# Joins, norm sums and roots moved between places of a hand-written order: attention by chunks, a maxout layer and a routed expert layer on one core

## The chip, the cores and the metric

One core of a Trainium2 chip runs the whole program. The metric is device microseconds of one execution. The engines are TensorE (PE, with its weight loads PEld), VectorE (DVE), ScalarE (ACT), GpSimd (POOL) and SyncE (SP), which here only issues DMAs. Each engine takes its instructions in the order in which the program issues them, and waits on semaphores that the others raise.

## The reference, cut to what matters

There are three stages, one after the other. The inputs are `q, k, v, a_re, a_im` of 4 x 8 x 768 x 48.

```python
mag = np.sqrt(a_re * a_re + a_im * a_im)
scale = np.minimum(mag, 0.999) / (mag + 1e-06)
a_re_n, a_im_n = (a_re * scale, a_im * scale)
for t in range(S):
    ar, ai = (a_re_n[:, :, t, :, None], a_im_n[:, :, t, :, None])
    new_re = ar * S_re - ai * S_im
    new_im = ar * S_im + ai * S_re
    kv = np.einsum('bhd,bhe->bhde', k[:, :, t], v[:, :, t])
    S_re, S_im = (new_re + kv, new_im)
    y[:, :, t] = np.einsum('bhd,bhde->bhe', q[:, :, t], S_re)
...
h = np.maximum(np.maximum(x @ w1, x @ w2), x @ w3)      # x: 3072 x 384, w: 384 x 768
x2 = h @ w_out
...
# each token of x2 goes to one of 8 experts by cosine with expert_emb:
out[mask] = gate_w[mask, None] * (np.maximum(x2[mask] @ e1[e], 0.0) @ e2[e])
```

## The kernel before, in words

**Chunks and pairs.** The 3072 tokens are 24 chunks of 128 (NC = 24), six to a batch. Two chunks make a pair g (12 pairs). For a pair the running products of the complex decay `a` are needed. They lie in one of four ring slots, and are made in this order: the decay is normalised in two halves m = 2g and 2g+1 (24 "norms"); GpSimd multiplies along blocks of 16 steps (`chain_steps(g, 1..15)`); VectorE joins the four blocks with three `join(g, b)`; GpSimd takes the pair's end for the state (`turns(g)`); ScalarE copies the pair's products into `z_t` (`stage_z(n)`), once for each chunk. Pair 0 is made by VectorE alone, in blocks of eight with seven joins. Pairs 0 and 1 come from memory directly. From pair 2 on a norm's result is stored to a scratch in memory, and loaded back from there into the ring (`store_unit`, `load_ring` on SyncE).

**One norm** is passed between ScalarE and VectorE: `norm_square` (ACT, L663), `norm_m2` (DVE, L1032), `norm_mag` (ACT, two activations, L668 and L670), `norm_sum` (DVE, L1037), `norm_rsqrt` (ACT, three activations, L674, L676, L679), `norm_inverse` (DVE, two operations, L1052 and L1054), `norm_rest` (ACT, L689), `norm_apply` (DVE, two operations, L1059 and L1062). There is one tile for the squares of all norms, so `norm_square(m)` waits for `norm_m2(m-1)`.

**The chunk loop** stands once for each engine, as an order written out by hand. In round n TensorE makes the scores of chunk n (L1627), turns its keys (L1637), adds to the state (L1648) and makes the answers (L1660, L1668). Among these it makes, for chunk n-1, the six groups of nine matmuls of the maxout layer (`moe_up`, `mm` of L1570, L1571, L1574), and for chunk n-2 the transposes of h and the product with `w_out` (`moe_ht`, `moe_down`). Its order in a round is: half the scores, `moe_ht(n-2, 0)`, the other scores, group 0, `moe_ht(n-2, 1)`, `moe_down(n-2)`, keys, group 1, state, group 2, answers, groups 3 to 5. Group 0 needs `x_hi` (ACT, L741) and `moe_max(n-2, 1, 1)`; group 3 needs `moe_max(n-1, 0, 1)`, group 4 `moe_max(n-1, 0, 2)`, group 5 `moe_copy(n-1, 1)` (ACT, L735). The scores of chunk n+1 need `k_decay(n+1)` (L1178).

VectorE prepares the next chunk in the same round: `z_norm(n+1)` (L1152), after ScalarE's `z_square(n+1)` (L709); `z_newton(n+1)` (two operations, L1159 and L1161), after ScalarE's `z_recip(n+1)` (two activations, L714 and L716); then `q_decay` and `k_decay`. Among these stand the maxima (`moe_max`, L1109), the mask (L1121), the state's turn (`rotation`, L1131 to L1136), `add_state` (L1146), the joins (four operations each, L1089 to L1093) and the norms. Which norms and joins a round has is set by `norms_in`, `joins_early` and `joins_late`.

ScalarE's order in a round is: `moe_x_hi(n-1)`, `moe_h_hi(n-2, 0)`, the square of a second norm, `stage_z(n+1)`, `moe_h_hi(n-2, 1)`, `z_square(n+1)`, `moe_copy(n-1, 0)`, `moe_out`, `kp_copy(n)`, `z_recip(n+1)`, all `norm_mag`, all `norm_rsqrt`, the next norm's square, `y_copy(n)`, `moe_copy(n-1, 1)`, all `norm_rest`. With `late_z` the staging stands after `kp_copy`.

After chunk 23 come the routing and the 30 expert tiles, which the change doesn't touch.

## Time and profile before

| | |
|---|---|
| median of 3 runs | 990.97 us (989.76 to 991.07) |
| the profiled execution | 990.71 us |
| its span, first to last instruction | 989.0 us |
| mean granted TensorE clock | 0.943 of full |
| busy share of the span | PE 88%, PEld 78%, DVE 66%, POOL 50%, ACT 47% |
| chain that ended last | PE 52%, DVE 17%, POOL 11%, ACT 6%, issue 5%, DMA 5%, SPq 2% |

Between the span and the profiled execution's time lie 1.7 us of start and end. The granted clock has two levels, full (2.4 GHz) and half (1.2 GHz); a value between them is a mean over a stretch that had both. The chunk loop takes the stretch from 65 to 645 us.

### The profile page before, as it was taken

To read this page: it belongs to the slowest core of one execution; us is meant where nothing else is said; L and a number is where in the kernel's file an instruction comes from. 1 tells how busy PE (TensorE), PEld (TensorE's weight loads), DVE (VectorE), ACT (ScalarE), POOL (GpSimd) and SP (SyncE) were. 2 spreads that over 40 slices of the span, in tenths; PEclk is the share of its full clock that TensorE was granted. 3 is DMA by queue.
4 is the path that set the end of the run, shared out by engine and by line. 5 is a ranking of instruction groups with operands and counts; after the bars stand their busy time and mean duration, and the time that the engine had idled before them with its cause. 6 is when DMAs were issued, how large, how long until landed. Compare 5 with 4: busy or idle time off the path is not lost.

```text
span 989.0 us, 18419 instructions
## 1 busy us (share of the span) xinstructions
PE 873.7 (88%) x6398; PEld 776.1 (78%) x6399; DVE 656.4 (66%) x1054; ACT 461.2 (47%) x859; POOL 491.1 (50%) x888
## 2 busy tenths in 40 slices
PE   0568887999989999999999999839999999999995
PEld 0445777888878898889889888838888888888785
DVE  5968677898799989999876755267323252556721
ACT  5765635555555566565344442233222242446521
POOL 1290998199998989889791000023222222223221
PEclk9767889999989999999999999967999999999998
DMA  9204232542414243331321110334411151416311
GB/s 302 65 20 106 73 81 68 139 106 71 118 53 112 87 118 87 93 86 54 87 64 40 38 46 19 139 137 167 168 40 40 40 168 40 167 34 210 121 40 32
DMA packets 42247, 90.80 MB, mean 92 GB/s; under 512 B 6312, under 2 KB 23728, under 8 KB 40768
## 3 DMA queue, kind: packets, MB, share of 16 engines
q1 hardware_dynamic: 38080, 77.48, 26.1%
q0 software_dynamic: 4096, 12.40, 4.0%
q8 instruction: 41, 0.67, 0.3%
q14 instruction: 30, 0.25, 0.1%
HBM read 70.20 MB, written 18.48 MB: 90 GB/s over the span
## 4 chain that ended last, share of the span: by engine, by line
PE 52%; DVE 17%; POOL 11%; ACT 6%; issue 5%; DMA 5%; SPq 2%; DVEq 0%; ACTq 0%; POOLq 0%
PE mm L1570 6%; PE mm L1574 5%; PE mm L1571 5%; PE yu L1570 4%; PE tr L1570 4%; PE tr L1571 4%; PE tr L1574 4%; PE yu L1571 4%; PE yu L1574 4%; POOL c_im L1889 3%; PE mm L1808 3%; POOL c_re L1888 3%; POOL ring L1891 2%; POOL ring L1892 2%; PE sc L1627 2%
## 5 line engine op out<-in xcount | busy, mean ns | idle before, releaser
L1570 PE MATMUL mm<-up_hi,x_hi 128*128 128x384 f32 x432 | 160.0, 370 | 34.2 <-DVE h_sb L1109 12.1
L1888 POOL TENSOR_TENSOR c_re<-ring 112x128 f32<-112x128 f32 x165 | 102.4, 620 | 108.0 <-DMA ring<-an_scratch 60.1
L1571 PE MATMUL mm<-up_lo,x_hi 128*128 128x384 f32 x432 | 149.9, 347 | 0.0
L1966 POOL DMA_INDIRECT out_rows<-g_o,rows_out x30 | 34.7, 1155 | 182.0 <-DVE g_o L1487 182.0
L1570 PEld LDWEIGHTS mm<-up_hi,x_hi 128*128 128x128 f32 x432 | 83.5, 193 | 50.6 <-DVE h_sb L1109 15.5
L952 ACT ACTIVATE g_h<-tr 128x512 f32<-128x512 f32 x60 | 35.8, 597 | 171.6 <-PE tr L1574 166.1
L1889 POOL TENSOR_TENSOR c_im<-ring 112x128 f32<-112x128 f32 x165 | 109.3, 662 | 0.0
L1574 PE MATMUL mm<-up_hi,x_lo 128*128 128x384 f32 x432 | 101.8, 345 | 0.0
L1891 POOL TENSOR_TENSOR ring<-c_re,c_im 112x64 f32<-112x64 f32 x165 | 83.8, 508 | 12.9
L1892 POOL TENSOR_TENSOR ring<-c_re,c_im 112x64 f32<-112x64 f32 x165 | 86.8, 526 | 0.0
L1109 DVE TENSOR_TENSOR h_sb<-mm,h_sb 128x384 f32<-128x384 f32 x96 | 52.9, 551 | 48.5 <-PE mm L1574 46.4
L1571 PEld LDWEIGHTS mm<-up_lo,x_hi 128*128 128x128 f32 x432 | 84.2, 195 | 0.0
L1478 DVE TENSOR_TENSOR gh_lo<-mm,gh_hi 128x512 fp32r<-128x512 f32 x60 | 41.4, 691 | 63.3 <-ACT gh_hi L960 60.8
L1570 PE MATMUL yu<-e_hi,gh_hi 128*128 (+1 forms) x240 | 83.0, 346 | 0.1
L1574 PEld LDWEIGHTS mm<-up_hi,x_lo 128*128 128x128 f32 x432 | 81.2, 197 | 0.0
L1571 PE MATMUL yu<-e_lo,gh_hi 128*128 (+1 forms) x240 | 80.9, 337 | 0.0
L1570 PE MATMUL tr<-e_hi,gx_hi 128*128 (+1 forms) x180 | 72.9, 405 | 2.0 <-DVE e_lo L1347 1.4
L1571 PE MATMUL tr<-e_lo,gx_hi 128*128 (+1 forms) x180 | 72.3, 402 | 0.0
L1627 PE MATMUL sc<-q_t,k_t 48*128 48x128 f32 x768 | 60.7, 303 | 11.5 <-DVE k_t L1178 9.1
L1627 PEld LDWEIGHTS sc<-q_t,k_t 48*128 48x128 f32 x768 | 51.5, 205 | 22.0 <-issue 22.0
L1347 DVE TENSOR_TENSOR e_lo<-raw,e_hi (+2 forms) x40 | 56.0, 1434 | 9.6 <-ACT e_hi L940 9.6
L1487 DVE TENSOR_SCALAR g_o<-yu,table_gate 128x384 f32 (+1 forms) x30 | 18.5, 618 | 63.9 <-PE yu L1574 63.3
(242 smaller groups left out, 2093.2 us busy)
## 6 DMA issues: line engine op xcount, KB each, us to landing
raw<-in_moe_w SPq DMA_DIRECT2D x16, 1536.0 KB
a_dn<-in_a_laid SPq DMA_DIRECT2D x20, 384.0 KB, 7.2
an_scratch<-a_dn SPq DMA_DIRECT2D x20, 384.0 KB, 2.3
ring<-an_scratch SPq DMA_DIRECT2D x20, 384.0 KB, 6.2
q_in<-in_q_laid SPq DMA_DIRECT2D x24, 224.0 KB, 3.0
k_in<-in_k_laid SPq DMA_DIRECT2D x24, 224.0 KB, 3.2
v_in<-in_v_laid SPq DMA_DIRECT2D x24, 192.0 KB, 3.3
x_scratch<-x_sb SPq DMA_DIRECT2D x24, 192.0 KB, 2.7
```

Of the source, the lines that this page charges most:

```text
L952: nc.scalar.activation(g_h[:, half * FREE:(half + 1) * FREE], tr[:, half, :], ACT.Relu) \
L1109: nc.vector.tensor_tensor(hh, mm[:, (3 * half + w) % 2, 0:FH], hh, ALU.max).then_inc(p_maxed, 1)
L1347: nc.vector.tensor_tensor(flat(lo), flat(raw), flat(hi).bitcast(F32), ALU.subtract).then_inc(expert_lo, 1)
L1478: nc.vector.tensor_tensor(gh_lo[:, part, :], mm[:, half, :].rearrange("p (k t) -> p k t", t=P), gh_hi[:, part, :].bitcast(F32), ALU.subtra ...
L1570: nc.tensor.matmul(out, hi[:, x, :], w_hi(x), start=(x == 0), stop=False)
L1571: nc.tensor.matmul(out, hi[:, x, :], w_lo(x), start=False, stop=False)
L1574: last = nc.tensor.matmul(out, lo[:, x, :], w_hi(x), start=False, stop=(x == K - 1))
L1627: last = nc.tensor.matmul(sc[:, b, h * P:(h + 1) * P], k_t[rows, x, h, :], q_t[n % 2][rows, x, h, :], start=(x == 0), stop=(x == 1))
L1888: nc.gpsimd.tensor_tensor(c_re[:, 0:count, :, :], cur, bc(prev[:, :, 0, :], 2, 2), ALU.mult).then_inc(chain_prod, 1)
L1889: nc.gpsimd.tensor_tensor(c_im[:, 0:count, :, :], cur, bc(prev[:, :, 1, :], 2, 2), ALU.mult).then_inc(chain_prod, 1)
L1891: nc.gpsimd.tensor_tensor(cur[:, :, 0, :], c_re[:, 0:count, 0, :], c_im[:, 0:count, 1, :], ALU.subtract).then_inc(chain_step, 1)
L1892: nc.gpsimd.tensor_tensor(cur[:, :, 1, :], c_re[:, 0:count, 1, :], c_im[:, 0:count, 0, :], ALU.add).then_inc(chain_step, 1)
```

## The change

It moves work within the orders of ScalarE and VectorE; no arithmetic is added or left out.

- Norm 10 goes from chunk 3 to chunk 4, which so has norms 10 and 11.
- Pair 2's joins: the first from ahead of `z_norm(3)` in chunk 2 to the end of that chunk, the second the same way into chunk 3, and the third from the end of chunk 2 into chunk 3. Pair 5's first join goes from the end of chunk 7 into chunk 8.
- In chunk 3 ScalarE stages chunk 4's products after `kp_copy`, as it does in chunk 1.
- In chunk 1 the state's turn and the second norm's first step stand behind the joins.
- `norm_sum` of every chunk goes ahead of `z_newton` and `moe_max(n-1, 0, 2)`.
- Norms 4 and 5, ahead of the loop and in chunk 0: their first steps, magnitudes and sums come earlier, their roots are apart, and their inverses stand between the scalings of chunk 0.

```diff
--- before.py
+++ after.py
@@ -472,16 +472,18 @@
 
             if n == 0:
                 return ()
-            first = 6 if n == 1 else n + 6 if n < 4 else n + 7
-            count = 2 if n in (1, 3) else 1
+            first = 6 if n == 1 else n + 6 if n < 5 else n + 7
+            count = 2 if n in (1, 4) else 1
             return tuple(m for m in range(first, first + count) if m < NORMS)
 
         joins_early = {1: [(1, b) for b in range(NBLK - 1)]}
         joins_late = {}
-        for g in range(DIRECT, NG):
-            joins_early[2 * g - 2] = [(g, 0), (g, 1)] if g < 5 else [(g, 1)]
+        joins_late[2] = [(2, 0)]
+        joins_early[3] = [(2, 1), (2, 2)]
+        for g in range(3, NG):
+            joins_early[2 * g - 2] = [(g, 0), (g, 1)] if g < 6 else [(g, 1)]
             joins_late[2 * g - 2] = [(g, 2)]
-            if g >= 5:
+            if g >= 6:
                 joins_late[2 * g - 3] = [(g, 0)]
 
         def router_bank(r):
@@ -831,19 +833,19 @@
             split_dn()
             norm_square(4, norm_of(4))
             low_copy(range(4, 8))
+            norm_square(5, norm_of(5))
+            norm_mag(4, norm_of(4))
             stage_z(0)
             z_square(0)
-            norm_square(5, norm_of(5))
+            norm_mag(5, norm_of(5))
             z_recip(0)
-            norm_mag(4, norm_of(4))
-            norm_mag(5, norm_of(5))
             low_copy(range(8, 12))
 
             for n in range(NC + 2):
                 prev, prev2, now, more = 1 <= n <= NC, n >= 2, n < NC, n + 1 < NC
                 norms = norms_in(n) if now else ()
                 later = norms_in(n + 1) if now else ()
-                late_z = n == 1
+                late_z = n in (1, 3)
                 if prev:
                     moe_x_hi(n - 1)
                 if prev2:
@@ -856,6 +858,8 @@
                     moe_h_hi(n - 2, 1)
                 if more and not late_z:
                     z_square(n + 1)
+                if n == 0:
+                    norm_rsqrt(4, norm_of(4))
                 if prev:
                     moe_copy(n - 1, 0)
                 if prev2:
@@ -866,13 +870,13 @@
                     kp_copy(n)
                 if n == 0:
                     low_copy(range(12, 14))
-                    norm_rsqrt(4, norm_of(4))
-                    norm_rsqrt(5, norm_of(5))
                 if more and late_z:
                     stage_z(n + 1)
                     z_square(n + 1)
                 if more:
                     z_recip(n + 1)
+                if n == 0:
+                    norm_rsqrt(5, norm_of(5))
                 for m in norms:
                     norm_mag(m, norm_of(m))
                 if n == 0:
@@ -1214,16 +1218,18 @@
             norm_apply(2, norm_of(2))
             first_chain(7)
             norm_apply(3, norm_of(3))
-            for number in range(7):
+            for number in range(4):
                 join(0, number)
             norm_m2(4, norm_of(4))
+            for number in range(4, 7):
+                join(0, number)
+            norm_m2(5, norm_of(5))
+            norm_sum(4, norm_of(4))
             z_norm(0)
-            norm_m2(5, norm_of(5))
+            norm_sum(5, norm_of(5))
             z_newton(0)
             q_decay(0)
             k_decay(0)
-            norm_sum(4, norm_of(4))
-            norm_sum(5, norm_of(5))
 
             for n in range(NC + 2):
                 prev, prev2, now, more = 1 <= n <= NC, n >= 2, n < NC, n + 1 < NC
@@ -1247,24 +1253,32 @@
                     moe_h_lo(n - 2, 1)
                 if now:
                     mask(n)
-                if now and n >= 1:
+                if now and n >= 2:
                     rotation(n)
-                for m in norms[1:]:
+                for m in norms[1:] if n >= 2 else ():
                     norm_m2(m, norm_of(m))
                 for g, number in joins_early.get(n, ()):
                     join(g, number)
+                if n == 1:
+                    rotation(n)
+                    for m in norms[1:]:
+                        norm_m2(m, norm_of(m))
                 if more:
                     z_norm(n + 1)
+                if n == 0:
+                    norm_inverse(4, norm_of(4))
                 if prev:
                     moe_max(n - 1, 0, 1)
                 if now:
                     add_state(n)
+                for m in norms:
+                    norm_sum(m, norm_of(m))
                 if more:
                     z_newton(n + 1)
                 if prev:
                     moe_max(n - 1, 0, 2)
-                for m in norms:
-                    norm_sum(m, norm_of(m))
+                if n == 0:
+                    norm_inverse(5, norm_of(5))
                 if more:
                     q_decay(n + 1)
                     k_decay(n + 1)
@@ -1273,8 +1287,6 @@
                 for m in norms:
                     norm_inverse(m, norm_of(m))
                 if n == 0:
-                    for m in (4, 5):
-                        norm_inverse(m, norm_of(m))
                     for m in (4, 5):
                         norm_apply(m, norm_of(m))
                 if prev:
```

## Rows read from the trace of the kernel before

**Rows 1.** The page: its first line, the span and the instructions.

```profile
span 989.0 us, 18419 instructions
```

**Rows 2.** By stretch: length, busy PE, PEld, DVE, ACT, POOL; clock, DMA share, GB/s.

```profile
114.77:148.12 33.35, 28.45 (x199) 25.61 (x199) 23.97 (x36) 12.93 (x26) 30.91 (x62) 0.75 0.37 99
148.12:176.44 28.32, 23.30 (x199) 20.83 (x199) 21.36 (x36) 16.97 (x34) 21.36 (x46) 0.94 0.19 60
176.44:202.73 26.29, 23.22 (x199) 20.52 (x198) 22.82 (x38) 12.38 (x26) 9.36 (x14) 0.94 0.52 132
202.73:224.47 21.74, 21.37 (x200) 19.54 (x199) 18.96 (x29) 13.57 (x27) 20.25 (x39) 0.99 0.49 121
224.47:269.04 44.57, 41.13 (x365) 37.03 (x365) 37.68 (x58) 25.23 (x51) 41.66 (x76) 1.00 0.36 95
269.04:319.26 50.22, 45.07 (x397) 41.26 (x397) 44.02 (x69) 25.58 (x52) 44.79 (x81) 0.93 0.31 84
319.26:340.87 21.61, 21.24 (x200) 19.40 (x199) 20.77 (x33) 12.84 (x26) 20.36 (x33) 1.00 0.25 79
471.97:496.37 24.40, 22.84 (x199) 20.91 (x198) 19.80 (x32) 9.58 (x20) 18.18 (x35) 0.93 0.36 88
```

**Rows 3.** VectorE timeline: start, duration, line, operation, count, [idle before, its releaser].

```profile
133.14 0.69 DVE L1089 TENSOR_TENSOR l_re<-ring 112x512 f32<-112x512 f32 x1 [5.38 <-POOL ring L1892]
...
271.17 0.69 DVE L1089 TENSOR_TENSOR l_re<-ring 112x512 f32<-112x512 f32 x1 [5.14 <-POOL ring L1892]
```

**Rows 4.** Timelines of VectorE and ScalarE near 49 us.

```profile
49.40 0.49 DVE L1089 TENSOR_TENSOR l_re<-ring 112x256 f32<-112x256 f32 x1
...
49.76 0.88 ACT L663 ACTIVATE n_sq<-a_dn 128x768 f32<-128x768 f32 x1
```

**Rows 5.** ScalarE timeline in chunk 3.

```profile
155.46 0.84 ACT L663 ACTIVATE n_sq<-a_dn 128x768 f32<-128x768 f32 x1 [3.10 <-DVE n_m L1032]
...
158.20 0.47 ACT L752 ACTIVATE h_hi<-tr 128x384 fp32r<-128x384 f32 x1
```

**Rows 6.** Timeline of TensorE in chunks 2 and 3.

```profile
139.64 0.69 PE L1570 MATMUL mm<-up_hi,x_hi 128*128 128x384 f32 x1 [3.69 <-DVE h_sb L1109]
...
146.34 0.44 PE L1570 MATMUL mm<-up_hi,x_hi 128*128 128x384 f32 x1 [0.85 <-ACT h_sb L735]
...
158.72 0.69 PE L1570 MATMUL mm<-dn_hi,h_hi 128*128 128x392 f32 x1 [3.38 <-ACT h_hi L752]
```

**Rows 7.** Timeline of VectorE in chunk 10.

```profile
325.13 1.28 DVE L1121 TENSOR_TENSOR att<-sc,causal 128x512 f32<-128x512 f32 x2
...
328.30 0.80 DVE L1089 TENSOR_TENSOR l_re<-ring 112x512 f32<-112x512 f32 x1
...
330.96 0.81 DVE L1152 SCALAR_TENSOR_TENSOR n<-z_sq 112x512 f32<-112x512 f32 x1
...
333.13 0.69 DVE L1159 SCALAR_TENSOR_TENSOR z_tmp<-n,z_sq 112x512 f32<-112x512 f32 x1 [0.43 <-ACT z_sq L716]
...
335.54 0.54 DVE L1166 TENSOR_TENSOR q_in<-q_in,z_tmp 112x256 f32<-112x256 f32 x1
...
339.27 0.81 DVE L1089 TENSOR_TENSOR l_re<-ring 112x512 f32<-112x512 f32 x1
...
342.99 1.23 DVE L1109 TENSOR_TENSOR h_sb<-mm,h_sb 128x384 f32<-128x384 f32 x2
```

**Rows 8.** Timeline of ScalarE in chunks 10 and 11.

```profile
333.54 0.61 ACT L670 ACTIVATE n_la<-n_la,log_col 128x384 f32<-128x384 f32 x1
...
343.62 0.51 ACT L741 ACTIVATE x_hi<-x_raw 128x384 fp32r<-128x384 f32 x1
```

**Rows 9.** Timeline of TensorE in chunks 6, 11 and 17.

```profile
244.87 0.45 PE L1570 MATMUL mm<-up_hi,x_hi 128*128 128x384 f32 x1 [1.95 <-ACT h_sb L735]
...
344.27 0.42 PE L1570 MATMUL mm<-up_hi,x_hi 128*128 128x384 f32 x1 [0.67 <-DVE h_sb L1109]
...
475.88 0.48 PE L1570 MATMUL mm<-up_hi,x_hi 128*128 128x384 f32 x1 [1.19 <-DVE h_sb L1109]
```

## Prediction

> **What bounds the kernel now.** I read the stretches first, cut where the scores of a chunk begin, so that each row is one round of the loop or two. A settled round is 21.6 us with TensorE busy for 21.2 of them [rows 2]: there TensorE is the bound and nothing else can shorten it. Longer are chunks 2, 3 and 4 (33.4, 28.3, 26.3 us), and chunks 8 and 9 together (50.2 for two). The timeline tells why. VectorE stood 5.38 us before the first join of pair 2 and 5.14 us before the first join of pair 5, both for GpSimd's chain [rows 3]; behind the first of these TensorE stood 3.69 us, then 0.85 us, and had 5.85 us of two groups that later take 1.78 each [rows 6]. In chunk 3 ScalarE stood 3.10 us for a norm's first step with the staging and a copy of h queued behind it [rows 5], and TensorE stood 3.38 us for that copy [rows 6]. The third view is one settled even chunk on VectorE and ScalarE [rows 7, 8], because it shows how near these two are to the path: group 0 of chunk 11 started 0.67 us late, behind VectorE's tail and the `x_hi` that follows it [rows 8, 9].
>
> **Start, chunks 0 and 1.** `norm_m2(4)` now stands ahead of the fifth of the seven joins. That join began at 49.40, but the squares of norm 4 are ready at 49.76 + 0.88 = 50.64 [rows 4]: VectorE waits 1.2 and spends 0.6, so pair 0 and chunk 0's staging come 1.8 later. The two sums ahead of `z_newton(0)` add 0.4, an estimate. In chunk 0 the roots of norm 5 no longer hold up `z_recip(1)`, which gives back most of it. Working both orders through the queues I leave 0.8 us of loss at the scores of chunk 2, with bounds of 2.2 (nothing comes back) and a gain of 1.0. Norms 4 and 5 are stored at about the same time as before: the first inverse's earlier place is spent by SyncE, whose stores stand behind the later copies of `y_end`. In chunk 1 the turn behind the joins costs nothing: staging waits there for `kp_copy`, so VectorE has a hole.
>
> **Chunk 2: gain 6.8.** With the first join behind `k_decay(3)`, VectorE goes on to `z_norm(3)` at 127.8 (133.14 - 5.38). Its work up to `k_decay(3)` then ends near 138.8, some three us ahead of TensorE. Gone are 3.69, 0.85 and the half-clock part of two groups, 5.85 - 2 x 1.78 = 2.3 [rows 6]: 6.8. The join that is now late needs GpSimd's chain, which ended at 133.1 while VectorE stood still. VectorE is now busy beside it; were GpSimd to run at half pace through that stretch, it would end at 127.8 + 2 x 5.4 = 138.5 [rows 3], still in time. The Trainium skill, SBUF — State Buffer, section "Who interferes with whom", says that a VectorE operation with two inputs in SBUF and a GpSimd operation that reads SBUF shut each other out; by it the half pace is to be feared here, and the last of the rivals below is what would follow.
>
> **Chunk 3: gain 1.0.** Norm 10's wait and its 3.38 us of TensorE go. But two joins stand ahead (2 x 2.66, from 328.30 to 330.96 [rows 7]), the staging can begin only behind them, and `z_norm(4)` behind the staging. Staging takes 1.9 (156.30 to 158.20 [rows 5]); for `z_square` I take 1.1 to 1.4, an estimate (1024 elements to a partition, where 384 take 0.51 [rows 8]): VectorE stands 3.3 us. Counted from the scores as in chunk 10: to the mask's end 7.15 (326.41 - 319.26); turn 1.9; joins 5.3; staging and square 3.3; `z_norm` 0.8; until the sum's end 2.95 (below); newton and maximum 2.0; decays 3.8 [rows 2, 7]. That is 27.3, against 28.3. TensorE stands about 2 us before group 3 and 3 us before group 4.
>
> **Chunk 4: loss 2.5.** It now has norms 10 and 11, so the square of norm 11 waits for `norm_m2(10)` and holds the staging and the copy of h, as in chunk 3 before: that copy began 10.1 us after the scores (158.20 - 148.12 [rows 2, 5]). With one norm less to apply I take 9.2. From its end VectorE needs h_lo 0.55, mask and turn 3.1 (325.13 to 328.30 [rows 7]), first step 0.55, two joins 4.3 (5.3 beside a busy GpSimd as in chunk 10; 4.3 is an estimate for an idle one, which waits for its ring here), `z_norm` 0.65, two magnitudes and the last sum 4.1 (2.95 below and 1.15 for the second magnitude), newton and maximum 2.0, decays 3.8: 19.1, and with 0.5 for the copy 28.8, against 26.3.
>
> **Chunk 5: loss 3.0.** The tail of chunk 4 holds a join and two inverses. In chunk 10 group 0 could start 5.0 us after the decays, with one inverse (339.27 to 344.27 [rows 7, 9]); a second (342.99 less its start at 341.9) adds 1.15. The scores follow the decays by 0.3 and group 0 could follow the scores by 2.7 (343.60 - 340.87 [rows 2, 9]): TensorE stands 3.1 us. 21.7 becomes 24.7.
>
> **The sum's new place: loss 5.9.** This is the part that repeats. In a chunk with an early join VectorE, not TensorE, sets when `z_norm` runs. It ended at 331.77; maximum and `add_state` followed, and newton started at 333.13, on ScalarE's reciprocal; q_decay at 335.54, that is 3.77 later [rows 7]. The magnitude is ready only at 333.54 + 0.61 = 334.15 [rows 8], 2.4 after `z_norm`. Put ahead of newton, the sum ends 2.95 after `z_norm`; newton (1.5) and maximum (0.5) follow, and q_decay starts 4.95 after: 1.18 later. The tail shifts with it, and group 0 of the next chunk, already 0.67 late, starts 1.85 late. ScalarE's roots start 0.9 earlier, but nothing on the path waits for them. In odd chunks `add_state` is held by TensorE past the magnitude, and the move is free. Chunks 6, 10, 12, 14 and 16 pay: 5 x 1.18 = 5.9. The price is zero only if the tail has cover; the 0.67 shows that it has none.
>
> **Chunks 8 and 9: gain 2.5.** The wait of 5.14 and its join leave chunk 7. Chunk 8 has two early joins: scores to end of decays is 20.1 in chunk 10 (339.3 - 319.2), and with 2.66 and 1.18 more 23.9; chunk 9 is 21.6 and 2.2 of wait at its group 0. That is 47.7, against 50.2 [rows 2].
>
> **Sum of waits:** 0.8 - 6.8 - 1.0 + 2.5 + 3.0 + 5.9 - 2.5 = +1.9.
>
> **The clock.** A wait of 1.19 us in chunk 17 was followed by half clock: that chunk took 24.40, which is 1.6 more than 21.6 + 1.19 [rows 2, 9]. The waits of 0.67 and 1.95 were not [rows 9]. The change puts waits of 1.7 to 3.1 at group 0 of chunks 5, 7, 9, 11, 13 and 15, where there were none over 1.1, and chunk 17's has paid already. I take three falls of these six, halfway between the two kinds of row: 3 x 1.6 = 4.8. The Trainium skill, TensorE: Matmul & The Clock Gate, section "What's actually happening", says that "the default state is throttled, and activity releases the throttle"; by it the work around a wait decides and not the wait alone, which fits both rows and would allow any number from none to six.
>
> **Sum:** the profiled execution took 990.7 us (span 989.0 [rows 1] and 1.7 around it), 0.3 below the median. 990.7 + 1.9 + 4.8 = 997.4. This is my forecast.
>
> **The rivals.**
>
> *The early chunks keep their gain (faster).* The mechanism is chunks 3 to 5: together 76.3 us before [rows 2], 80.8 in my sum. If VectorE's queue fits as well as before, through shorter joins or the staging finding its data early, they take 76 or less, and 4.8 more of chunk 2's gain is kept; with no fall of the clock that gives 990.7 + 1.9 - 4.8 = 987.8. For it: the stands of 5.38 and 5.14 were real losses, and the change removes both. Against it: each of the three chunks gets work in front of its decays. It decides, with the clock held, from chunks 3 to 5 at 77 us or less together (990.7 + 1.9 - 3.8 = 988.8).
>
> *The clock holds (no change).* My waits without falls give 990.7 + 1.9 = 992.6. For it stands the wait of 1.95 with full clock behind it.
>
> *The clock falls every time (slower).* Six falls: 990.7 + 1.9 + 9.6 = 1002.2. For it stand 1.19, and 3.69 with half speed right behind it.
>
> *A join of pair 2 still waits (slower).* If GpSimd ends its chain over 1 us later than my bound, the late join holds norm 8's inverse and the maxima of group 4 behind it. At 3 us it gives 990.7 + 1.9 + 4.8 + 3 = 1000.4.
>
> **How the numbers follow.** Forecast (two to four falls, 994 to 1000) 0.42; clock holds 0.16; falls every time or a waiting join 0.14; faster 0.28, since my sums of new waits in chunks 3 to 5 are longer than any row and every one of them can be too large. A measurement of this kernel tells a change of about 0.2% (2.0 us, 989.0 to 993.0) from none. Faster 0.28, within 0.2% 0.16, slower 0.56 (0.42 and 0.14). Both signs hold much of it, so the range is wide: from 986, a little under the faster rival, to 1002, at the clock's worst, which leaves about 2 in 10 outside. The forecast's own range is 994 to 1000.
>
> **What would show each step.** Right: no stand on GpSimd at the first joins of pairs 2 and 5; scores of chunk 3 near 142; VectorE standing some 3 us before `z_norm(4)`; ScalarE standing for a norm's first step in chunk 4; `norm_sum` of even chunks waiting near 1.4 us for the magnitude; waits of 1.7 to 2.3 at group 0 of odd chunks; several chunks with a granted clock below 1.00. Wrong: odd chunks from 11 on still 22.3 us, or chunks 3 to 5 within 77 us; then the time falls below the one before. It would also be wrong if group 0's wait were bound by `x_hi`'s DMA and not by the tail.

## The result and the profile after

The change makes the kernel slower: 994.07 us median of 20 runs (990.82 to 999.28) against 989.77 us of 20 runs of the kernel before (988.37 to 992.02); the ratio is 1.0040, 95% interval 1.0027 to 1.0053. The forecast was 997.4 us, its range 986 to 1002. The runs after lie over 8.5 us where those of before lie over 3.7. The profiled execution took 994.46 us, its span 992.7 us. One run of the kernel before, in the comparison of the last experiments, took 2854.72 us and is left out of every number below.

The stretches of the kernel after, cut as in [rows 2] where the scores of a chunk begin; the rows are chunks 1 to 5, chunks 6 and 7, chunks 8 and 9, and chunks 10 to 13, 15 and 17:

```profile
82.05:110.81 28.76, 25.30 (x193) 20.77 (x193) 21.66 (x37) 16.86 (x31) 12.38 (x22) 0.88 0.41 108
110.81:133.87 23.06, 21.55 (x200) 19.35 (x199) 19.48 (x30) 13.61 (x27) 21.52 (x41) 1.00 0.53 145
133.87:168.40 34.53, 26.93 (x199) 24.29 (x199) 25.74 (x41) 13.56 (x27) 32.14 (x62) 0.80 0.17 51
168.40:196.93 28.53, 23.32 (x200) 20.84 (x199) 22.01 (x35) 15.37 (x31) 17.56 (x31) 0.94 0.37 91
196.93:222.45 25.52, 22.85 (x199) 20.91 (x198) 22.84 (x36) 14.28 (x28) 23.91 (x43) 0.93 0.51 134
222.45:269.65 47.20, 42.58 (x366) 38.64 (x365) 40.11 (x61) 26.00 (x52) 43.62 (x80) 0.96 0.32 90
269.65:317.96 48.31, 44.44 (x397) 40.31 (x397) 41.60 (x66) 25.38 (x51) 36.89 (x65) 0.96 0.32 88
317.96:339.57 21.61, 21.24 (x200) 19.40 (x199) 19.75 (x31) 12.97 (x26) 20.20 (x37) 1.00 0.25 79
339.57:363.10 23.53, 21.27 (x199) 19.39 (x199) 21.81 (x35) 12.98 (x26) 17.48 (x32) 1.00 0.42 107
363.10:382.83 19.73, 19.36 (x168) 17.71 (x167) 17.84 (x28) 12.89 (x26) 18.48 (x33) 1.00 0.27 86
382.83:406.66 23.83, 21.27 (x199) 19.39 (x199) 22.11 (x35) 12.98 (x26) 18.81 (x34) 1.00 0.42 106
428.27:451.66 23.39, 21.27 (x200) 19.39 (x199) 21.68 (x35) 12.97 (x26) 18.85 (x34) 1.00 0.36 91
473.31:498.62 25.31, 22.85 (x200) 20.92 (x199) 20.76 (x33) 9.62 (x20) 18.29 (x34) 0.93 0.34 84
```

Read against [rows 2]: chunk 2 fell from 33.35 to 23.06 us, and chunk 3 grew from 28.32 to 34.53. Chunks 4 and 5 grew by 2.2 and 3.8. From the scores of chunk 2 to those of chunk 6 the kernel before took 109.70 us (224.47 - 114.77) and the one after 111.64 (222.45 - 110.81): the gain of chunk 2 was spent before chunk 6 began. From there to the scores of chunk 18, 271.90 us became 276.17 (498.62 - 222.45), 4.3 more. The two spans differ by 3.7 us (992.7 - 989.0): the scores of chunk 2 came 4.0 earlier than before (110.81 against 114.77), chunks 2 to 5 took 1.9 more, chunks 6 to 17 4.3 more, and what follows them 1.5 more.

The timeline of GpSimd and VectorE after, at pair 2's first join in its new place:

```profile
135.12 0.32 POOL L1904 TENSOR_TENSOR ring<-c_re,c_im 112x64 f32<-112x64 f32 x1
135.47 0.69 DVE L1093 TENSOR_TENSOR l_re<-ring 112x512 f32<-112x512 f32 x1 [3.47 <-POOL ring L1904]
```

The stand of 5.38 us in [rows 3] did not go away; it moved by one place and became 3.47 us. TensorE's side, ten of its waits at maxout groups after, all for VectorE's maxima (the first is group 0 of chunk 3, the second and third are groups 3 and 4 of chunk 3, the others group 0 of chunks 5, 7, 9, 11, 13, 15 and 17):

```profile
140.35 0.42 PE L1582 MATMUL mm<-up_hi,x_hi 128*128 128x384 f32 x1 [3.75 <-DVE h_sb L1113]
157.62 0.44 PE L1582 MATMUL mm<-up_hi,x_hi 128*128 128x384 f32 x1 [1.62 <-DVE h_sb L1113]
162.41 0.69 PE L1582 MATMUL mm<-up_hi,x_hi 128*128 128x384 f32 x1 [1.86 <-DVE h_sb L1113]
...
201.96 0.42 PE L1582 MATMUL mm<-up_hi,x_hi 128*128 128x384 f32 x1 [2.30 <-DVE h_sb L1113]
249.15 0.41 PE L1582 MATMUL mm<-up_hi,x_hi 128*128 128x384 f32 x1 [2.21 <-DVE h_sb L1113]
297.47 0.42 PE L1582 MATMUL mm<-up_hi,x_hi 128*128 128x384 f32 x1 [1.43 <-DVE h_sb L1113]
344.19 0.41 PE L1582 MATMUL mm<-up_hi,x_hi 128*128 128x384 f32 x1 [1.89 <-DVE h_sb L1113]
387.75 0.41 PE L1582 MATMUL mm<-up_hi,x_hi 128*128 128x384 f32 x1 [2.19 <-DVE h_sb L1113]
432.75 0.41 PE L1582 MATMUL mm<-up_hi,x_hi 128*128 128x384 f32 x1 [1.75 <-DVE h_sb L1113]
478.13 0.41 PE L1582 MATMUL mm<-up_hi,x_hi 128*128 128x384 f32 x1 [2.09 <-DVE h_sb L1113]
```

The stretch from behind the second of these waits (1.62 us) nearly to the end of chunk 3, in the form of [rows 2], had half clock throughout:

```profile
158.10:168.20 10.10, 8.24 (x26) 7.56 (x25) 7.44 (x11) 5.19 (x11) 9.48 (x18) 0.50 0.03 6
```

From chunk 5 on each odd chunk's group 0 stands 1.4 to 2.3 us, where chunk 11 stood 0.67 in [rows 9]. The cause is on VectorE in the chunk ahead. This is chunk 10 after, against [rows 7]:

```profile
329.56 0.94 DVE L1156 SCALAR_TENSOR_TENSOR n<-z_sq 112x512 f32<-112x512 f32 x1
...
332.93 0.62 DVE L1041 SCALAR_TENSOR_TENSOR n_m<-n_la,n_m 128x384 f32<-128x384 f32 x1 [1.49 <-ACT n_la L672]
333.47 0.94 DVE L1163 SCALAR_TENSOR_TENSOR z_tmp<-n,z_sq 112x512 f32<-112x512 f32 x1
...
335.52 0.62 DVE L1170 TENSOR_TENSOR q_in<-q_in,z_tmp 112x256 f32<-112x256 f32 x1
```

The sum (L1041) stands 1.49 us for the magnitude, with newton (L1163) queued behind it. From `z_norm`'s end (330.50) to q_decay it is 5.02 us, and it was 3.77.

### The profile page after: what moved, and what is told of

Its sections match the earlier page's. It is cut to its first block, busy times and chain, and to the rows that moved or that the text cites. A ratio compares the mean times of both kernels' runs of the same rounds, so it can differ in the third digit from the quotient of the medians.

```text
span 992.7 us, 18419 instructions
## 1 busy us (share of the span) xinstructions
PE 872.8 (88%) x6398; PEld 776.7 (78%) x6399; DVE 658.2 (66%) x1054; ACT 462.5 (47%) x859; POOL 495.0 (50%) x888
## 4 chain that ended last, share of the span: by engine, by line
PE 55%; DVE 19%; issue 8%; ACT 8%; DMA 4%; POOL 4%; SPq 1%; DVEq 0%; ACTq 0%; POOLq 0%
PE mm L1582 7%; PE mm L1586 6%; PE mm L1583 6%; PE yu L1582 4%; PE tr L1582 4%; PE tr L1586 4%; PE tr L1583 4%; PE yu L1583 4%; PE yu L1586 4%; PE mm L1820 3%; PE sc L1639 2%; DVE l_im L1094 2%; DVE l_re L1093 2%; PE yu L1680 2%; DVE h_sb L1113 1%
## 5 line engine op out<-in xcount | busy, mean ns | idle before, releaser
L1900 POOL TENSOR_TENSOR c_re<-ring 112x128 f32<-112x128 f32 x165 | 99.0, 600 | 102.2 <-DMA ring<-an_scratch 54.0
L1978 POOL DMA_INDIRECT out_rows<-g_o,rows_out x30 | 34.6, 1155 | 181.7 <-DVE g_o L1499 181.7
L1901 POOL TENSOR_TENSOR c_im<-ring 112x128 f32<-112x128 f32 x165 | 117.9, 714 | 0.0
L1586 PE MATMUL mm<-up_hi,x_lo 128*128 128x384 f32 x432 | 103.8, 350 | 0.0
L1639 PE MATMUL sc<-q_t,k_t 48*128 48x128 f32 x768 | 57.9, 294 | 13.3 <-DVE k_t L1182 10.9
L1639 PEld LDWEIGHTS sc<-q_t,k_t 48*128 48x128 f32 x768 | 49.1, 196 | 23.4 <-issue 23.4
```

The lines of the kernel that those rows point to most:

```text
L1586: last = nc.tensor.matmul(out, lo[:, x, :], w_hi(x), start=False, stop=(x == K - 1))
L1639: last = nc.tensor.matmul(sc[:, b, h * P:(h + 1) * P], k_t[rows, x, h, :], q_t[n % 2][rows, x, h, :], start=(x == 0), stop=(x == 1))
L1900: nc.gpsimd.tensor_tensor(c_re[:, 0:count, :, :], cur, bc(prev[:, :, 0, :], 2, 2), ALU.mult).then_inc(chain_prod, 1)
L1901: nc.gpsimd.tensor_tensor(c_im[:, 0:count, :, :], cur, bc(prev[:, :, 1, :], 2, 2), ALU.mult).then_inc(chain_prod, 1)
```

## The experiments

All twelve kernels differ from the one before or the one after only in the order of the same operations; each computes the whole of the reference. Of each kernel there is one trace, so what a stretch took is read from a single execution, and what a change is worth from the medians.

**The sums back behind the second maximum**, all else as changed:

```diff
-                for m in norms:
-                    norm_sum(m, norm_of(m))
                 if more:
                     z_newton(n + 1)
                 if prev:
                     moe_max(n - 1, 0, 2)
+                for m in norms:
+                    norm_sum(m, norm_of(m))
```

> The changed kernel with norm_sum of chunks 1 to 16 put back behind the second maximum, all else as changed. Theory A (the prediction's): the sum ahead of newton holds VectorE about 1.2 us in each even chunk and lengthens the wait at group 0 of the next odd chunk, and the longer waits bring the half clock. Then chunks 6 to 17 get back 5 to 7 us of waits and most of the falls (1.6 us each): 984 to 987 us, below both kernels; group 0 of chunk 11 waits 0.7 us again and not 1.9. Rival B: the waits of the odd chunks come from the joins and norms of the new placing, and the sum is free: 993 to 995 us, group 0 of chunk 11 still 1.9 us late.

Measured: 984.58 us (982.63 to 986.70, 6 runs), ratio to before 0.9940, interval 0.9919 to 0.9962. Theory A. The rest of the change is thus a gain, and the sums' place cost 9.5 us (994.07 - 984.58). Stretches of this kernel: chunks 8 and 9 together, then chunks 11, 13 and 17:

```profile
268.42:315.07 46.65, 42.99 (x398) 38.73 (x397) 42.69 (x66) 25.26 (x51) 43.23 (x76) 1.00 0.33 91
336.68:359.03 22.35, 21.27 (x200) 19.39 (x199) 20.21 (x33) 12.76 (x26) 18.97 (x35) 1.00 0.46 113
379.35:402.05 22.70, 21.29 (x200) 19.40 (x199) 20.45 (x34) 12.96 (x26) 19.05 (x35) 1.00 0.43 112
467.60:490.78 23.18, 21.27 (x200) 19.40 (x199) 20.28 (x33) 9.54 (x20) 18.21 (x34) 1.00 0.38 93
```

Chunks 11 and 13 are 1.18 and 1.13 us shorter than after the change, and the clock is full in all four rows. From the scores of chunk 6 to those of chunk 18 this trace is 9.1 us shorter than the one after the change (267.11, from 223.67 to 490.78, against 276.17), so nearly all of the 9.5 us lies there.

**The sums ahead of newton alone**, in the kernel before:

```diff
+                for m in norms:
+                    norm_sum(m, norm_of(m))
                 if more:
                     z_newton(n + 1)
                 if prev:
                     moe_max(n - 1, 0, 2)
-                for m in norms:
-                    norm_sum(m, norm_of(m))
```

> The kernel before with nothing changed but norm_sum put ahead of newton and the second maximum. Theory A: slower than before by 5 to 7 us of waits in chunks 7, 9, 11, 13, 15 and 17, and by up to 5 falls of the clock at 1.6 us: 995 to 1002 us, with more spread between executions. Rival B: no change, 989 to 991 us.

Measured: 996.48 us (993.69 to 998.98, 6 runs), ratio 1.0059, interval 1.0036 to 1.0083. So this one move costs 6.6 us by itself (996.48 - 989.90, the median of before in this comparison). Its chunks 7, 9, 11 and 13:

```profile
248.45:273.91 25.46, 22.87 (x199) 20.94 (x199) 22.20 (x34) 12.97 (x26) 23.72 (x45) 0.93 0.38 99
295.53:319.41 23.88, 21.29 (x199) 19.41 (x198) 21.80 (x35) 12.92 (x26) 19.42 (x36) 1.00 0.42 106
341.02:366.27 25.25, 22.85 (x199) 20.92 (x198) 22.11 (x35) 12.95 (x26) 20.58 (x37) 0.93 0.38 100
386.03:411.33 25.30, 22.84 (x199) 20.92 (x198) 21.59 (x35) 12.94 (x26) 19.18 (x33) 0.93 0.40 100
```

TensorE stood 2.21 us at group 0 of chunk 7 and 2.22 at group 0 of chunk 9. The clock fell behind the first and not behind the second, and the chunks differ by 1.6 us (25.46 - 23.88). In chunk 11 it fell here after 2.03, and in chunk 13 of the kernel after the change it held after 2.19. Pair 5's first join, which stood 5.14 us in the kernel before, stood 0.21 here, because VectorE came to it later, and chunk 8 took 21.6 us in place of 28.5: in the kernel before, this wait hides a part of what the sums' place costs.

**Pair 5's first join alone**, in the kernel before:

```diff
-            joins_early[2 * g - 2] = [(g, 0), (g, 1)] if g < 5 else [(g, 1)]
+            joins_early[2 * g - 2] = [(g, 0), (g, 1)] if g < 6 else [(g, 1)]
-            if g >= 5:
+            if g >= 6:
```

> The kernel before with nothing changed but the first join of pair 5 moved from the end of chunk 7 into chunk 8. Theory A: the wait of 5.14 us for GpSimd goes, with 4.28 us of TensorE and the half clock behind it; a second early join in chunk 8 gives back some 2.7 us: chunks 8 and 9 take 46 to 47.5 us in place of 50.2, 986 to 987.5 us in all. Rival C: the join is only done later, and GpSimd's next pairs wait for it: 989 to 991 us.

Measured: 988.62 us (985.77 to 991.19, 12 runs), ratio 0.9987, interval 0.9973 to 1.0001. Chunks 8 and 9 took 47.4 us in its trace against 50.22 before [rows 2]; the median shows 1.3 us of these 2.8, and the interval just takes in no change at all.

**The start with chunks 0 and 1 alone**: the first two rounds of ScalarE's and VectorE's orders as changed, all else as before.

```diff
-                if now and n >= 1:
+                if now and n >= 2:
                     rotation(n)
...
+                if n == 0:
+                    norm_inverse(4, norm_of(4))
```

> The kernel before with only the new order of norms 4 and 5 ahead of the loop and in chunk 0, and the turn of chunk 1 behind the joins. The prediction's sum: 0.8 us later at the scores of chunk 2, and 990 to 991 us in all. Rival D, read from the changed kernel's trace: the scores of chunk 2 start 4.0 us earlier, but chunk 2 still waits for GpSimd's chain of pair 2, whose data land 1.6 us earlier; so about 1.6 us are left at the scores of chunk 3: 987.5 to 988.5 us.

Measured: 989.64 us (986.84 to 992.39, 12 runs), ratio 0.9999, interval 0.9984 to 1.0015: nothing. Its VectorE and TensorE in chunk 2:

```profile
132.94 0.69 DVE L1091 TENSOR_TENSOR l_re<-ring 112x512 f32<-112x512 f32 x1 [9.14 <-POOL ring L1902]
```
```profile
139.43 0.69 PE L1580 MATMUL mm<-up_hi,x_hi 128*128 128x384 f32 x1 [8.72 <-DVE h_sb L1111]
```

The join starts at 132.94, in the kernel before at 133.14 [rows 3], though the scores of chunk 2 came 1.3 us earlier (113.47). VectorE reached it earlier and stood 9.14 us in place of 5.38. That need not be the new start's doing: VectorE stood 8.62 us at this join in the kernel with pair 5's join alone, which has the old start, and the join started there at 132.98. As long as this join stands ahead of `z_norm(3)`, GpSimd's chain sets the time, and whatever is won in front of it is lost there.

**All three joins of pair 2 early in chunk 3**, with the sums behind the maximum:

```diff
-        joins_late[2] = [(2, 0)]
-        joins_early[3] = [(2, 1), (2, 2)]
+        joins_early[3] = [(2, 0), (2, 1), (2, 2)]
```

> The kernel with the sums put back (984.6 us), and the first join of pair 2 not at the end of chunk 2 but ahead of the other two in chunk 3. There VectorE stood 3.76 us for GpSimd's chain in front of this join, and TensorE 3.30 us at group 0 of chunk 3. Theory A (the waiting join costs, as the last rival of the prediction said, and was the dearest wait left in chunks 2 and 3): the wait at group 0 of chunk 3 is gone, 3.3 us and the half clock behind it, and 2.7 of it come back as a third early join ahead of z_norm(4): 982.5 to 984. Rival B (the length of VectorE's queue in chunk 3 bounds, not the wait): z_norm(4) stays where it was plus 2.7, no gain at all, 984.6 to 987.5.

Measured: 984.58 us (983.57 to 986.51, 5 runs), ratio 0.9954, interval 0.9940 to 0.9968: no difference from the kernel it came from (984.58, interval 0.9919 to 0.9962) that these runs can tell. The stand at the join is gone, and chunk 3 fell from 32.39 to 30.67 us, but TensorE then stood 5.38 us at its group 3, since the joins ahead of `z_norm(4)` are now three, and chunk 6 grew by 1.2. The wait was removed, and nothing was won by it that the medians show. Rival B.

**Norm 10 back in chunk 3**, with the sums behind the maximum:

```diff
-            first = 6 if n == 1 else n + 6 if n < 5 else n + 7
-            count = 2 if n in (1, 4) else 1
+            first = 6 if n == 1 else n + 6 if n < 4 else n + 7
+            count = 2 if n in (1, 3) else 1
```

> The kernel with the sums put back (984.6 us), and norm 10 in chunk 3 again, so that chunk 4 has one norm and chunk 3 two. Theory A (the second norm costs in chunk 4 what the prediction said, 2.5 us there and 1 to 3 in chunk 5, and in chunk 3, where ScalarE now stages late, its first step holds only itself and a copy of h): chunk 4 falls from 30.7 to about 27, chunk 5 from 22.7 to 21.7, chunk 3 grows from 32.4 by at most 2: 981 to 983. Rival B (the norm costs the same wherever it stands, some 3.4 us of TensorE behind the copy of h): 984 to 986. If it comes out above 986, the move of norm 10 was worth its place.

Measured: 981.48 us (980.14 to 986.36, 5 runs), ratio 0.9922, interval 0.9896 to 0.9947. Chunks 3, 4 and 5 of this kernel:

```profile
135.70:170.27 34.57, 26.53 (x199) 23.50 (x199) 28.23 (x45) 17.38 (x34) 32.28 (x60) 0.84 0.16 49
170.27:197.18 26.91, 25.70 (x200) 23.12 (x199) 21.94 (x35) 12.35 (x25) 13.93 (x25) 0.83 0.48 128
197.18:219.73 22.55, 21.28 (x200) 19.41 (x199) 19.93 (x32) 13.49 (x27) 21.06 (x40) 1.00 0.50 117
```

Chunk 4 fell from 30.7 to 26.9 and chunk 3 grew by 2.2, as theory A had it. The median is 3.1 us lower than with norm 10 in chunk 4, but the two intervals overlap: this points to a gain and doesn't settle it.

**Pair 2 and norm 10 as before**, with the start and pair 5's join as changed and the sums behind the maximum; the previous edit, and:

```diff
-        joins_late[2] = [(2, 0)]
-        joins_early[3] = [(2, 1), (2, 2)]
-        for g in range(3, NG):
+        for g in range(DIRECT, NG):
...
-                late_z = n in (1, 3)
+                late_z = n == 1
```

> The kernel with the sums put back, and pair 2 and norm 10 as in the kernel before: what is left of the change is the start with chunks 0 and 1, and pair 5's first join. Theory A (the parts about add up, and the start's gain is swallowed by the wait for GpSimd's chain as long as pair 2's first join stands ahead of z_norm(3)): 989.9 less 0.2 for the start less 1.3 for pair 5's join, 988.4, with the join of pair 2 waiting 7 to 9 us; the moves of pair 2 and norm 10 are then worth 3.8 us. Rival B (the start brings its 4 us by itself, and the moves of pair 2 bring nothing): 984.5 to 985.5.

Measured: 989.65 us (985.96 to 995.12, 10 runs), ratio 1.0009, interval 0.9990 to 1.0028. Theory A. The first join of pair 2 stood 9.56 us for GpSimd again and chunk 2 took 34.38 us. What the change wins, it wins through pair 2: 989.65 - 984.58 = 5.1 us, with intervals that don't touch. The kernel with norm 10 back in chunk 3 (981.48) differs from this one only in pair 2's joins and chunk 3's late staging: these are worth 989.65 - 981.48 = 8.2 us, again with intervals that don't touch, and norm 10's new place takes some 3 of them back.

**The sums in the middle**, between newton and the second maximum, all else as changed:

```diff
-                for m in norms:
-                    norm_sum(m, norm_of(m))
                 if more:
                     z_newton(n + 1)
+                for m in norms:
+                    norm_sum(m, norm_of(m))
                 if prev:
                     moe_max(n - 1, 0, 2)
```

> The changed kernel with the sums between z_newton and the second maximum, and not ahead of both. Theory A (what costs in the changed kernel is that the sum waits for the magnitude with z_newton behind it; behind z_newton the magnitude is ready, and the order against the maximum is free): as with the sums put back, 984.6, within 1.5 us; group 0 of chunks 11, 13 and 15 waits 0.7 to 1.1 us, and the clock stays full there. Rival B (any place ahead of the second maximum makes TensorE's group 4 late, and the clock falls as in the changed kernel): 990 to 995, with waits of 1.7 to 2.2 us at group 0 of these chunks or 0.5 us or more at group 4.

Measured: 980.47 us (979.60 to 980.80, 4 runs), ratio 0.9904, interval 0.9887 to 0.9920. It is 13.6 us under the changed kernel, by swapping two neighbours in VectorE's queue. Chunk 10 on its VectorE:

```profile
323.25 0.81 DVE L1156 SCALAR_TENSOR_TENSOR n<-z_sq 112x512 f32<-112x512 f32 x1
...
325.42 0.69 DVE L1163 SCALAR_TENSOR_TENSOR z_tmp<-n,z_sq 112x512 f32<-112x512 f32 x1 [0.43 <-ACT z_sq L718]
...
326.90 0.55 DVE L1041 SCALAR_TENSOR_TENSOR n_m<-n_la,n_m 128x384 f32<-128x384 f32 x1
...
327.84 0.41 DVE L1170 TENSOR_TENSOR q_in<-q_in,z_tmp 112x256 f32<-112x256 f32 x1
```

The sum doesn't stand, and q_decay follows `z_norm` by 3.78 us, as in the kernel before. It is also better than the place behind the maximum, by 4.1 us in the medians, which theory A had not expected. The copy of h for group 5 stands behind ScalarE's roots, and these behind the sum. TensorE at group 5 of chunk 8, first with the sums behind the maximum and then with them in the middle:

```profile
290.90 0.44 PE L1582 MATMUL mm<-up_hi,x_hi 128*128 128x384 f32 x1 [2.17 <-ACT h_sb L737]
```
```profile
286.53 0.45 PE L1582 MATMUL mm<-up_hi,x_hi 128*128 128x384 f32 x1 [1.02 <-ACT h_sb L737]
```

From the scores of chunk 8 to those of chunk 18 that is worth 1.9 us (490.78 - 268.42 against 485.23 - 264.74). What else divides the two traces lies mostly ahead of chunk 4, where the time of the first scores alone differs by 2.8 us (70.21 and 67.41), so the rest of the 4.1 is not split further.

**The sums in the middle alone**, in the kernel before:

```diff
                 if more:
                     z_newton(n + 1)
-                if prev:
-                    moe_max(n - 1, 0, 2)
                 for m in norms:
                     norm_sum(m, norm_of(m))
+                if prev:
+                    moe_max(n - 1, 0, 2)
```

> The kernel before with one line moved: the sums between z_newton and the second maximum, not behind it. Ahead of z_newton they cost 6.6 us (996.5 against 989.9). Theory A (behind z_newton they cost nothing, and the roots of ScalarE end 0.5 us sooner, with the copy of h for group 5 behind them, which TensorE waits for in chunks 6 and 8 with 2.0 and 2.2 us): 986 to 988.5. Rival B (no effect either way; the 4 us that the middle place brought against the last one came from the other edits or the start's luck): 989 to 990.5.

Measured: 987.75 us (985.96 to 990.08, 10 runs) against 989.61, ratio 0.9982, interval 0.9967 to 0.9996: a gain of some 1.9 us (0.4 to 3.3 by the interval) where the place ahead of newton lost 6.6. Theory A.

**The sums in the middle and norm 10 in chunk 3**, all else as changed; the sums as two kernels above, and:

```diff
-            first = 6 if n == 1 else n + 6 if n < 5 else n + 7
-            count = 2 if n in (1, 4) else 1
+            first = 6 if n == 1 else n + 6 if n < 4 else n + 7
+            count = 2 if n in (1, 3) else 1
```

> The changed kernel with two edits of it altered: the sums between z_newton and the second maximum (alone 980.5 us) and norm 10 in chunk 3 as before (with the sums behind the maximum 981.5 against 984.6 us). Theory A (the two places don't touch each other): 980.5 less 3.1, 977.4, within 1.5; chunk 4 near 27 and chunk 5 near 22. Rival B (both bring the same thing, the staging and the copy for group 5 of chunks 4 to 6 in time, so they don't add): 980 to 981.5.

Measured: 980.31 us (980.19 to 982.27, 4 runs), ratio 0.9909, interval 0.9881 to 0.9937. The two edits don't add up (980.5 with the first alone): rival B's number, but not for its reason. Chunk 4 took 23.9 us, 3 less than expected, and chunk 5 22.9, but chunk 3 took 36.1: VectorE stood 5.11 us at the join of pair 2, against 1.85 with the sums in the middle alone. GpSimd's chain had begun 1.7 us later in this execution (100.32 against 98.61) and ended 1.8 later, and VectorE reached the join 1.5 earlier.

**The same with all joins of pair 2 early in chunk 3:**

```diff
-        joins_late[2] = [(2, 0)]
-        joins_early[3] = [(2, 1), (2, 2)]
+        joins_early[3] = [(2, 0), (2, 1), (2, 2)]
```

> The same, and all three joins of pair 2 early in chunk 3. With the sums behind the maximum this last edit brought nothing (984.6 against 984.6 us): chunk 3 fell from 32.4 to 30.7 us and chunk 5 and one half-clock stretch gave it back. Theory A (the waiting join at the end of chunk 2 is not worth more than the 2.7 us that a third early join costs in chunk 3): as the kernel with these two edits alone, within 1.5 us. Rival B (the wait was the dearest left, and only the norms in chunk 4 hid its gain): 2 us or more under it.

Measured: 978.60 us (977.44 to 980.17, 4 runs), ratio 0.9887, interval 0.9858 to 0.9916. This is the fastest version by its median, 1.1% under the kernel before. It is 1.7 us under the previous kernel, between the two theories, and the intervals overlap. In the traces chunk 3 fell by 2.7 us (36.1 to 33.4) and chunk 4 took 1.3 more.

**The kernel with the sums in the middle and norm 10 in chunk 3, its start undone** (all edits ahead of the loop and in chunks 0 and 1, of which these are two):

```diff
-                if now and n >= 2:
+                if now and n >= 1:
                     rotation(n)
...
-                if n == 0:
-                    norm_inverse(4, norm_of(4))
```

> The kernel of the first edit pair (sums in the middle, norm 10 in chunk 3) with the start ahead of the loop and chunks 0 and 1 as in the kernel before. It prices the start where pair 2's first join is out of the way. The profile after the change had the scores of chunk 2 4.0 us earlier than before, where the prediction expected them 0.8 later. Theory A (the start brings its 3 to 4 us, and only the wait for GpSimd's chain ahead of z_norm(3) swallowed it when it was done alone, 989.6 against 989.9): 3 to 4 us slower than that kernel. Rival B (what moved the scores of chunk 2 was the time at which the first inputs landed, not the order): the same within 1 us. The prediction's own term would make it 0.8 faster.

Measured: 979.99 us (979.30 to 983.14, 4 runs), ratio 0.9910, interval 0.9879 to 0.9942; with the start 980.31. Rival B: the order of the start is worth nothing measurable here either. Over the kernels whose sums stand behind the maximum the scores of chunk 2 came at 114.77 and 112.84 us without the new start and at 112.46, 112.79, 113.47, 113.63 and 116.05 with it: the scatter is larger than any effect.

## Why the prediction came out as it did

The direction and the main cause were right. Taken apart by the medians, the change is: start and pair 5's join -0.2 us (989.65 - 989.88), pair 2 and norm 10 -5.1, the sums' place +9.5, together +4.2. (The three steps form one chain of kernels, so their sum is no test. Added to the kernel before, the sums' place alone cost 6.6 and not 9.5; the runs' spread allows the two to be equal, and the wait of pair 5 that it hid there would account for a difference.) The prediction had -1.7 (0.8 - 2.5), -2.3 (-6.8 - 1.0 + 2.5 + 3.0) and +10.7 (5.9 + 4.8), together +6.7. That +6.7 and +4.2 lie near each other is in part luck: the start and chunks 2 and 3 were off by 4.8 and 3.8 us in the trace, in opposite directions, and the prediction did not see that the one would take back the other.

- **The sum's new place: right, in mechanism and size.** Forecast: q_decay 4.95 us behind `z_norm`; measured 5.02. Forecast: 1.18 us for each group 0 behind an even chunk; chunks 11, 13 and 15 are 1.18, 1.13 and 1.06 us longer than with the sums put back. In the middle place the wait is gone and so is the price. One clause was wrong: that nothing on the path waits for ScalarE's earlier roots. Chunk 12 took 19.7 us where the kernel before took 20.7 (383.91 - 363.19), and the middle place, which has the earlier roots without the wait, beats the last place.
- **The clock: three falls of six, as taken, which is luck.** Chunks 5, 7 and 9 had half clock behind their wait (25.5, 25.4 and 24.7 us), and chunks 11, 13 and 15 had not. Three was a midpoint, not a derivation, and this is one execution; over the 20 runs the granted clock goes from 0.941 to 0.956, and in the kernel with the sums alone five of these six chunks fell. The sizes match too: chunk 13 with a wait of 2.19 and full clock took 23.83 us, and chunk 7 of the kernel with the sums alone, with 2.21 and a fall, 25.46. The Trainium skill, TensorE: Matmul & The Clock Gate, section "What's actually happening", says that the default is throttled and that activity releases the throttle. The equal waits with different outcomes agree with a rule on activity and not on the wait alone.
- **Chunks 2 and 3: the step that failed.** The prediction had 26.5 and 27.3 us (53.8; the terms shown for chunk 3 add up to 27.2) and the late join "still in time". Measured: 23.1 and 34.5 (57.6). GpSimd's chain ended at 135.44, inside the bound of 138.5. But VectorE was through with `k_decay(3)` at 132.0 and not at 138.8: the scores of chunk 2 came 4.0 us earlier, and VectorE's work from there to `k_decay(3)` took 2.8 less than in the sum. The last rival happened (it was priced at 3 us; VectorE stood 3.47 and TensorE 3.75), and its condition was put on the wrong side: not GpSimd late, but VectorE early. Of the 7.2 us that chunk 3 took over the sum, 4.4 are VectorE's: its decays ended 31.7 us after the chunk's scores (165.57 - 133.87), not 27.3. The other 2.8 passed between these decays and the scores of chunk 4, which TensorE reached at half clock; the prediction's clock term has no fall for chunk 3.

  The stand itself depends on which of the two comes when: the scores of chunk 2 came 4.8 us sooner than in the sum (0.8 later than before was forecast, and 4.0 sooner was measured), and those of chunk 4 still came at 168.4, near the 169.4 that the sum gives. In the six kernels that have this join ahead of `z_norm(3)`, VectorE came to it between 122.3 and 127.8 and stood 5.4 to 9.6 us, and the join started between 131.9 and 134.0 in all of them.

  Yet moving it was no mistake: pair 2's joins in their new places and the late staging are worth 8.2 us, against the 7.8 that the prediction had for chunks 2 and 3, and norm 10's new place costs some 3, against 5.5 for chunks 4 and 5 (989.65 - 981.48 and 984.58 - 981.48; the second is not settled, and the prediction's 1.0 for chunk 3 has norm 10's going in it).
- **GpSimd beside a busy VectorE.** From the first step of pair 2's chain to the end that the join waits for, GpSimd took 33.8 us before (99.29 to 133.10) and 37.8 after (97.65 to 135.44). All traces agree: where VectorE was busy for 19.5 to 20.8 us of this stretch the chain took 33.8 to 34.6 (six kernels), where it was busy for 28 it took 37.7 to 38.5 (six), and where it did not stand for the join at all, 39.1 and 40.3 (two). The Trainium skill, SBUF — State Buffer, section "Who interferes with whom", says that a VectorE instruction with two SBUF inputs contends with a GpSimd instruction that reads SBUF. The direction agrees, and the half pace feared for the whole stretch was not reached.
- **Start, chunks 0 and 1: not to be told from nothing.** Forecast a loss of 0.8, the trace after showed a gain of 4.0 at the scores of chunk 2, and alone it measured 0.0. The mechanism held ahead of chunk 1: in the five kernels with the old start the first scores come at 65.6 to 65.9 us and chunk 0 takes 16.8 to 18.1, in the nine with the new one they come at 66.7 to 70.2, later as forecast, and chunk 0 takes 14.8 to 16.4, which gives it back. Of the 4.0, 2.5 came in chunk 1 (28.8 us against 31.3) and 1.5 before it, which is inside the scatter: the scores of chunk 1 come at 82.4 to 83.8 with the old start and at 81.5 to 85.6 with the new. With the sums in the middle chunk 1 takes 28.1 to 29.6 us, with or without the new start, and with them behind the maximum 30.0 to 31.3, so the sums of its two norms have a part in it; with the sums ahead of newton alone it took 31.7, so they are not all of it.
- **Chunks 4 and 5: right.** 28.5 and 25.5 us against 28.8 and 24.7; without the fall in chunk 5, which the prediction counts apart, 25.5 is 23.9, with a stand of 2.30 us where 3.1 was forecast.
- **Chunks 8 and 9: right within 1 us by the traces.** After the whole change they took 48.3 us with a fall in chunk 9, so 46.7 without it, forecast 47.7. The forecast has 1.2 for the sum's new place in it; without that, 46.5 compares with 46.65 with the sums put back and 47.4 when done alone, with a granted clock of 0.94 in chunk 8. The median of the move alone gave only 1.3 us.

What stays open: why equal waits are sometimes followed by half clock and sometimes not, and how much of the 4.1 us between the two good places of the sums is the copy for group 5.

## What to carry to other kernels

In a queue that runs in order, an operation that depends on another engine goes behind the operations whose inputs are ready before its own, by measured ready times, and no further back: here swapping two neighbours was worth 13.6 us of 994, since the wait came back every second chunk, and one place further back was 4.1 us worse again. A join that waits for a slower engine gains nothing from being reached sooner. Putting it behind work that the next chunk needs first paid here (8.2 us with the moves around it), though it still stood 3.5 us there, and one place later still brought nothing that the medians show. No run here shortened GpSimd's chain. When a change bundles six edits, time them apart first: this one held a gain of 5 us and a loss of 9.5.

## What the runs showed that was not expected

- A stand of TensorE may cost more than its length, and its length does not say when. Of fourteen stands of 1.4 to 2.3 us at group 0 of the odd chunks 5 to 17, in the changed kernel and the one with the sums alone, nine were followed by a lower granted clock (0.93 in the chunk's row) and five were not; the difference is 1.6 us for a chunk. No stand at group 0 of chunks 7 to 17 with the sums put back, 0.7 to 1.5 us, was followed by one, but the stand of 1.19 us in chunk 17 of the kernel before was.
- The spread of a kernel's runs is not explained by these stands. It was 8.5 us over 20 runs of the changed kernel, but 9.2 us over 10 runs of the kernel with pair 2 and norm 10 as before, whose trace has no stand over 1.4 us at any group 0 of chunks 5 to 17.
- An earlier start of chunk 2 hardly reaches the end where pair 2's first join stands ahead of `z_norm(3)` (six kernels): the scores of chunk 2 come at 111.9 to 115.5 us there, and GpSimd's chain lets the join start at 131.9 to 134.0.
